# A fused attention and expert kernel: gates, own products and the last weight pieces take other places in the written order, and the late weight halves change engine

## What is computed

```
mag = sqrt(a_re^2 + a_im^2); scale = min(mag, 0.999) / (mag + 1e-6)
S = (a * scale) * S + outer(k[t], v[t])        # complex, per batch and head
y[t] = q[t] @ real(S)
xn = x / sqrt(mean(x^2) + 1e-6) * rms_g
x = (silu(xn @ w_gate) * (xn @ w_val)) @ w_out # 384 -> 1536 -> 384
expert = argmax(normalized(x) @ normalized(emb).T / tau)
out = gate * relu(x @ w1[expert]) @ w2[expert]
```

## Time and profile before

| | before |
|---|---|
| median of 3 runs | 1297.83 us (1294.12 to 1298.23) |
| profiled execution | 1298.23 us, span 1296.5 us |
| tensor engine busy | 1176.7 us, 91% |
| vector engine busy | 793.2 us, 61% |
| scalar engine busy | 616.1 us, 48% |
| GpSimd busy | 355.0 us, 27% |
| mean granted clock of the tensor engine | 0.977 |

### The profile page before, as it was taken

How to read it: one execution, slowest core, us unless ns; L and a number is a source line. 1 busy time by engine, 2 the same in 40 slices (tenths; PEclk the granted TensorE clock), 3 DMA queues, 4 the chain that set the end, 5 groups by cost and what they waited for, 6 DMA issues and landing times. The chain is left out here.

```text
span 1296.5 us, 46197 instructions
## 1 busy us (share of the span) xinstructions
PE 1176.7 (91%) x20003; PEld 1025.5 (79%) x20003; DVE 793.2 (61%) x1551; ACT 616.1 (48%) x1322; POOL 355.0 (27%) x345
## 2 busy tenths in 40 slices
PE   1778999899999999899999999899978999999995
PEld 0456879687887869687787969688848999999995
DVE  5886858586766858576675858444117555545553
ACT  4766463654636463564536374443322344333342
POOL 7131341333315041332405042300003132322221
PEclk9889999999999999999999999999998999999998
DMA  6221320210203020210203020000006633433310
GB/s 158 63 63 39 100 63 15 45 33 21 57 3 75 4 63 15 45 34 15 63 3 72 6 45 9 21 9 9 8 13 181 229 109 125 143 126 136 131 38 29
DMA packets 153380, 78.35 MB, mean 60 GB/s; under 512 B 130715, under 2 KB 144571, under 8 KB 153200
## 3 DMA queue, kind: packets, MB, share of 16 engines
q1 hardware_dynamic: 144800, 59.04, 17.2%
q0 software_dynamic: 4384, 11.88, 3.1%
q10 hardware_dynamic: 4016, 4.73, 1.0%
HBM read 66.15 MB, written 11.06 MB: 60 GB/s over the span
## 5 line engine op out<-in xcount | busy, mean ns | idle before, releaser
L965 PE MATMUL pO<-wo_sb,hid 128*128 128x384 f32 x576 | 207.3, 499 | 11.6 <-issue 11.0
L771 ACT ACTIVATE silu<-pGV 128x256 f32<-128x256 f32 x144 | 55.1, 383 | 260.6 <-PE pGV L953 260.1
L965 PEld LDWEIGHTS pO<-wo_sb,hid 128*128 128x128 f32 x576 | 104.0, 193 | 70.1 <-issue 15.5
L951 PE MATMUL pGV<-xT_hi,wg_hi 128*128 128x256 f32 x432 | 134.0, 310 | 0.7 <-DVE hid L619 0.4
L619 DVE TENSOR_TENSOR hid<-silu,pGV 128x256 f32<-128x256 f32 x144 | 58.5, 413 | 115.5 <-ACT silu L771 115.1
L1275 ACT ACTIVATE h_hi<-pH 128x256 fp32r<-128x256 f32 x128 | 49.1, 384 | 164.7 <-PE pH L1220 164.7
L952 PE MATMUL pGV<-xT_lo,wv_hi 128*128 128x256 f32 x432 | 121.6, 282 | 0.0
L953 PE MATMUL pGV<-xT_hi,wg_lo 128*128 128x256 f32 x432 | 121.6, 281 | 0.0
L951 PE MATMUL pGV<-xT_hi,wv_hi 128*128 128x256 f32 x432 | 121.6, 281 | 0.0
L952 PE MATMUL pGV<-xT_lo,wg_hi 128*128 128x256 f32 x432 | 121.5, 281 | 0.0
L953 PE MATMUL pGV<-xT_hi,wv_lo 128*128 128x256 f32 x432 | 121.5, 281 | 0.0
(11 more groups left out here) (230 smaller groups left out, 3081.9 us busy)
## 6 DMA issues: line engine op xcount, KB each, us to landing
w_sb<-in_moe_w SPq DMA_DIRECT2D x18, 1536.0 KB, 10.4
re<-in_a_re SPq DMA_DIRECT2D x24, 192.0 KB, 2.8
im<-in_a_im SPq DMA_DIRECT2D x24, 192.0 KB, 3.9
qin<-in_q SPq DMA_DIRECT2D x24, 192.0 KB, 2.8
kin<-in_k SPq DMA_DIRECT2D x24, 192.0 KB, 3.3
vin<-in_v SPq DMA_DIRECT2D x24, 192.0 KB, 3.7
routed_rows<-x ACTq DMA_DIRECT2D x24, 192.0 KB, 2.0
wo_sb<-in_moe_w_gate SPq DMA_DIRECT2D x3, 768.0 KB, 6.2
```

The costliest lines, as they stand in the source:

```text
L951: mm.matmul(to, hi, x_hi[:, kk, :], start=(kk == 0), stop=False)
L965: ins = mm.matmul(pO[:, 0:HD], hid[:, f, s_ * P:(s_ + 1) * P], wo_sb[:, f, :], start=(f == 0), stop=(f == NF - 1))
```

## The change

It has three parts. In `STEPS`, gate 2 stands ahead of the two squares and level 0 instead of behind level 0 and the route; own 0 stands ahead of gate 11 instead of behind level 6; sines 0, rotate 0 and own 1 stand right behind level 6, ahead of the first output parts. In `ONE_STEPS`, the four warm steps are gone; pieces 14 to 17 are done among the turns instead of among levels 0 to 2; every gate stands earlier, gates 0 and 1 ahead of level 0; own and sines stand in the places they have in `STEPS`, except that own 0 stands behind level 6. And the high and low halves of pieces 14 to 17 are made on the vector engine (`late_high`, `late_low`, with semaphores of their own), not on the scalar engine.

```diff
+ALL_PIECES, PIECES_AHEAD = 6 * KC, 14
 STEPS = [
...
-    ("lev", "turn", 10), ("lev", "turn", 11), ("lev", "first", 1), ("pre", "recip", 1), ("pre", "quotients", 1),
+    ("lev", "turn", 10), ("lev", "turn", 11), ("lev", "first", 1), ("pre", "recip", 1), ("pre", "quotients", 1), ("glu", "gate", 2),
     ("fin", "square", 0), ("fin", "square", 1),
-    ("lev", "level", 0), ("fin", "route", 0), ("glu", "gate", 2), ("glu", "gate", 3), ("pre", "tangent", 0), ("pre", "tangent", 1),
+    ("lev", "level", 0), ("fin", "route", 0), ("glu", "gate", 3), ("pre", "tangent", 0), ("pre", "tangent", 1),
...
-    ("lev", "level", 5), ("fin", "logits", 0), ("glu", "gate", 11),
-    ("lev", "level", 6), ("pre", "own", 0), ("finA", "out", 0), ("finA", "out", 1),
-    ("lev", "turn_back", 0), ("pre", "sines", 0), ("pre", "rotate", 0), ("pre", "own", 1), ("finA", "out", 2), ("lev", "turn_back", 1), ("pre", "sines", 1), ("pre", "rotate", 1), ("finA", "out", 3),
+    ("lev", "level", 5), ("fin", "logits", 0), ("pre", "own", 0), ("glu", "gate", 11),
+    ("lev", "level", 6), ("pre", "sines", 0), ("pre", "rotate", 0), ("pre", "own", 1), ("finA", "out", 0), ("finA", "out", 1),
+    ("lev", "turn_back", 0), ("finA", "out", 2), ("lev", "turn_back", 1), ("pre", "sines", 1), ("pre", "rotate", 1), ("finA", "out", 3),
 ONE_STEPS = [
+    ("lev", "turn", 0), ("lev", "turn", 1), ("glu", "norm", 0), ("wts", "late_high", 14), ("lev", "turn", 2), ("lev", "turn", 3), ("wts", "split", 14),
+    ("wts", "late_high", 15), ("lev", "turn", 4), ("lev", "turn", 5), ("glu", "scale", 0), ("wts", "late_low", 14),
+    ("wts", "late_high", 16), ("lev", "turn", 6), ("lev", "turn", 7), ("lev", "first", 0), ("wts", "split", 15), ("glu", "turn_in", 0),
+    ("wts", "late_high", 17), ("wts", "late_low", 15), ("lev", "turn", 8), ("lev", "turn", 9), ("wts", "split", 16), ("glu", "gate", 0), ("wts", "late_low", 16),
+    ("lev", "turn", 10), ("lev", "turn", 11), ("lev", "first", 1), ("next", "squares", 0), ("next", "squares", 1), ("wts", "split", 17), ("glu", "gate", 1), ("next", "signs", 0),
+    ("wts", "late_low", 17), ("next", "abs", 0), ("next", "abs", 1),
+    ("lev", "level", 0), ("next", "signs", 1), ("pre", "roots", 0), ("pre", "roots", 1), ("glu", "gate", 2), ("pre", "sums", 0),
+    ("lev", "level", 1), ("pre", "sums", 1), ("glu", "gate", 3), ("glu", "gate", 4), ("pre", "recip", 0),
+    ("lev", "level", 2), ("pre", "quotients", 0), ("glu", "gate", 5), ("glu", "gate", 6), ("pre", "recip", 1), ("pre", "quotients", 1),
+    ("lev", "level", 3), ("pre", "tangent", 0), ("pre", "tangent", 1), ("pre", "double", 0), ("pre", "double", 1), ("glu", "gate", 7), ("glu", "gate", 8),
+    ("lev", "level", 4), ("pre", "angle", 0), ("pre", "angle", 1), ("glu", "gate", 9), ("glu", "gate", 10),
+    ("lev", "level", 5), ("pre", "phase", 0), ("glu", "gate", 11),
+    ("lev", "level", 6), ("pre", "phase", 1), ("pre", "own", 0), ("pre", "own", 1), ("finA", "out", 0), ("finA", "out", 1),
+    ("lev", "turn_back", 0), ("pre", "sines", 0), ("pre", "rotate", 0), ("finA", "out", 2), ("lev", "turn_back", 1), ("pre", "sines", 1), ("pre", "rotate", 1), ("finA", "out", 3),
+    ("lev", "output", 0), ("lev", "output", 1), ("lev", "products", 0), ("lev", "state", 0), ("sq", "squares", 0), ("sq", "squares", 1),
+    ("finA", "out", 4), ("finA", "out", 5), ("sq", "signs", 0), ("sq", "signs", 1),
...
@@ sync
-                    sp.wait_ge(sm["wlo_ready"], 2 * 3 * KC)
+                    sp.wait_ge(sm["wlo_ready"], PIECES_AHEAD)
+                    sp.wait_ge(sm["wlo_late"], ALL_PIECES - PIECES_AHEAD)
@@ vector
+                            elif step == "late_high":
...
+                                dve.wait_ge(staged[n % 3], (n // 3 + 1) * 16)
+                                w.tensor_scalar((wg_hi, wv_hi)[n % 2][:, kk, part], landing[n % 3][:, kk, :], gcol[:, kk:kk + 1], None, ALU.mult
+                                                ).then_inc(sm["whi_late"], 1)
+                            elif step == "late_low":
...
+                                dve.wait_ge(sm["wdiff_ready"], x + 1)
+                                w.tensor_copy((wg_lo, wv_lo)[n % 2][:, kk, part], difference(x)).then_inc(sm["wlo_late"], 1)
@@ tensor, split
-                                pe.wait_ge(sm["whi_ready"], x + 1)
-                                if x > PIECES_AHEAD:
-                                    pe.wait_ge(sm["wlo_ready"], x)
-                                elif x >= 2:
+                                if x < PIECES_AHEAD:
+                                    pe.wait_ge(sm["whi_ready"], x + 1)
+                                else:
+                                    pe.wait_ge(sm["whi_late"], x + 1 - PIECES_AHEAD)
+                                if 2 <= x < PIECES_AHEAD:
                                     pe.wait_ge(sm["wlo_ready"], x - 1)
+                                elif x > PIECES_AHEAD:
+                                    pe.wait_ge(sm["wlo_late"], x - PIECES_AHEAD)
@@ tensor, gate
-                                    pe.wait_ge(sm["wlo_ready"], 2 * (f * 3 // NF + 1) * KC)
+                                    pe.wait_ge(sm["wlo_ready"], min(2 * (f * 3 // NF + 1) * KC, PIECES_AHEAD))
+                                if m == 0 and f == 2 * NF // 3:
+                                    pe.wait_ge(sm["wlo_late"], ALL_PIECES - PIECES_AHEAD)
```

More of the change, by code:

```diff
@@ L131 @@
 ONE_STEPS = [
[L132 to L145, removed]
@@ L146 @@
-    ("lev", "turn_back", 1), ("pre", "sines", 0), ("pre", "rotate", 0), ("finA", "out", 1), ("finA", "out", 2), ("lev", "output", 0), ("lev", "output", 1), ("pre", "sines", 1), ("pre", "rotate", 1), ("lev", "products", 0),
-    ("lev", "state", 0), ("sq", "squares", 0), ("sq", "squares", 1), ("finA", "out", 3), ("finA", "out", 4), ("finA", "out", 5), ("sq", "signs", 0), ("sq", "signs", 1),
+    ("lev", "turn", 0), ("lev", "turn", 1), ("glu", "norm", 0), ("wts", "late_high", 14), ("lev", "turn", 2), ("lev", "turn", 3), ("wts", "split", 14),
@@ L251, in build @@
             pM = ps(a, "pM", [P, 512])
-            names = ("wo_loaded a_cleared masks_ready scales_ready whi_ready wdiff_ready wlo_ready xhi_ready small_loaded sq_ready m2_ready turns_ready mag_ready a1_ready den_ready rm_ready "
+            names = ("wo_loaded a_cleared masks_ready scales_ready whi_ready wdiff_ready wlo_ready whi_late wlo_late xhi_ready small_loaded sq_ready m2_ready turns_ready mag_ready a1_ready den_ready rm_ready "
                      "signed_ready dd_ready rd_ready ima_ready rmd_ready t_ready r_ready rr_ready absre_ready at_ready th_ready "
@@ L279, in halves, with difference @@
                 return x[:, :, :].rearrange("p h t -> p (h t)").rearrange("p (n two l) -> p n two l", two=2, l=L)[:, :, side, :]
+            def difference(x):
+                return (pGV[x % 2] if x < PIECES_AHEAD else pO)[:, 0:THIRD]
             def pipeline(eng, body):
@@ L756, in body @@
                                 act.wait_ge(sm["wdiff_ready"], x + 1)
-                                s.activation((wg_lo, wv_lo)[n % 2][:, kk, part], (pGV[x % 2] if x < PIECES_AHEAD else pO)[:, 0:THIRD], ACT.Copy).then_inc(sm["wlo_ready"], 1)
+                                s.activation((wg_lo, wv_lo)[n % 2][:, kk, part], pGV[x % 2][:, 0:THIRD], ACT.Copy).then_inc(sm["wlo_ready"], 1)
                             elif step == "output" and x % 2:
@@ L813, in body @@
                                 pe.wait_ge(staged[n % 3], (n // 3 + 1) * 16)
-                                pe.wait_ge(sm["whi_ready"], x + 1)
-                                if x > PIECES_AHEAD:
-                                    pe.wait_ge(sm["wlo_ready"], x)
-                                elif x >= 2:
-                                    pe.wait_ge(sm["wlo_ready"], x - 1)
-                                mm.matmul((pGV[x % 2] if x < PIECES_AHEAD else pO)[:, 0:THIRD], times_g[kk], landing[n % 3][:, kk, :], start=True, stop=False)
-                                mm.matmul((pGV[x % 2] if x < PIECES_AHEAD else pO)[:, 0:THIRD], minus[:, :], (wg_hi, wv_hi)[n % 2][:, kk, part],
-                                          start=False, stop=True).then_inc(sm["wdiff_ready"], 1)
+                                if x < PIECES_AHEAD:
[3 more added lines that the diff above has]
+                                if 2 <= x < PIECES_AHEAD:
+                                    pe.wait_ge(sm["wlo_ready"], x - 1)
+                                elif x > PIECES_AHEAD:
+                                    pe.wait_ge(sm["wlo_late"], x - PIECES_AHEAD)
+                                to = difference(x)
+                                mm.matmul(to, times_g[kk], landing[n % 3][:, kk, :], start=True, stop=False)
+                                mm.matmul(to, minus[:, :], (wg_hi, wv_hi)[n % 2][:, kk, part], start=False, stop=True).then_inc(sm["wdiff_ready"], 1)
                             if step == "names_turned":
```

5 lines of the change are left out of this document (4 added, 1 removed).

## The result

| | before | after |
|---|---|---|
| median, 5 runs each on one chip | 1297.83 us (1292.96 to 1298.88) | 1305.91 us (1304.58 to 1310.14) |
| profiled execution | 1298.23 us, span 1296.5 | 1301.46 us, span 1299.6 |
| mean granted clock, profiled execution | 0.977 | 0.970 |

The ratio is 1.0079, with a 95% interval of 1.0051 to 1.0106. The time lies inside the range of the prediction, but the case it called likeliest, no difference, did not happen.

What follows compares the result with a forecast made beforehand. The tensor engine is fullest (68.6 of 73.3 us in a plain pass), so time lies in its idle places. Terms 3.6 - 6.0 + 3.6 = +1.2 on 1298.23 give 1299.4 us; range 1293.9 to 1301.7, wider 1290 to 1307.

Steps and rivals of the forecast that it cites:

- no difference: Whole kernel: time within 0.3%, 1293.9 to 1301.7 us, about what a measurement can't tell from no change; chance 0.50.
- Part 1, +3.6 us: Level 1, second chunk, plain passes: gate 2's multiply ahead in the vector queue delays it 0.4 us, nine times: +3.6 us.
- Part 2, -6.0 us: Outputs of passes 2 to 10: earlier own and sines remove the second chunk's output wait behind the state, -6.0 us.
- Part 3, +3.6 us: Pass 1: removed warming is spent on waiting, the vector engine's added copies delay level 0; +3.6 us, bounds -5.3 and +8.
- the walk: Pass 1 order followed with estimated lengths: level 0 on the vector engine near 123.4 against 115.17, level 6 7.3 us later.
- (a): Port, at the state's decay: both multiplies of rotate 1 hold it off, the wait stays, 6.0 us back, 1305.4; chance 0.10.
- (b): Clock in pass 1: three more half clock stretches, 1.7 us each, give +5 us, 1304.5; chance 0.22.
- (c): Pass 1 gains: the vector chain keeps up, so part 3 is -5.3 us, 1290.5; chance 0.13.
- (e): Part 1 in the plain passes costs nothing, the rest as forecast: 1295.8 us; chance 0.07.
- (d): Pauses where the second chunk's loads are issued move off: the 7.4 us before L928 gone, 1292.0; chance 0.08.

Runs made afterwards that it cites:

- e1_gate2: Kernel before with only gate 2 moved ahead of level 0 in the plain passes (part 1); ratio 1.0090 to before, median 1307.56 us.
- e2_own: Kernel before with only part 2: own 0 ahead of gate 11, sines 0, rotate 0 and own 1 right behind level 6; ratio 0.9948, median 1288.44 us.
- e4_one: Kernel before with only part 3: new pass 1 order and late weight halves on the vector engine; ratio 1.0012, median 1296.25 us.
- The filling matmul: Kernel before with part 1 plus one unused 128 x 384 matmul ahead of level 1 in every plain pass; ratio 1.0074 to before, median 1301.73 us.
- k4_one_order: Kernel before with part 3, but gate 1 and the last low half behind level 0 of pass 1; ratio 1.0002 to before, median 1293.37 us.

## Why the prediction was wrong, step by step

**Part 1, +3.6 us: the mechanism right, the term too small.** The place (level 1, second chunk), the cause (0.4 us in the vector queue), and the wait (1.34 us in pass 2; 11.2 us in the list of the kernel after, 12.4 in e1_gate2's) are as written. The step that failed is "level 1 starts about 0.4 us later [...] nine times: +3.6 us", with its upper bound of 0.5 for each: e1_gate2 is 12.5 us slower. 4.4 of them are the wait; up to 7.9 go with a granted clock of 0.9740 in place of 0.9801, with half clock granted right behind that wait in two of the nine passes. Pass 11, costed at nothing, has no such wait in e1_gate2 either. I had weighed the clock in pass 1 alone and priced a longer wait in passes 2 to 10 at its length. With 12.5 in place of 3.6 the sum would have been 1298.23 + 10.1 = 1308.3 us, against 1305.9 measured.

**Part 2, -6.0 us: right.** e2_own gave 0.9948, which is 6.7 us. The reduction fitted in its hole, the state's wait went, and the wait ahead of the first output part stayed (8.5, now 8.9; 9.9 in e2_own).

**Part 3, +3.6 us: the walk right in its places and too short for pass 1, the term not decided.** Level 0 on the vector engine was put between 122 and 125, and came at 121.67; counted from the pass's start that is 24.5 us against 15.0, 9.5 later where 8.2 was walked. The copies took 0.47 and 0.68 us (0.47 and 0.7 written), two of the splits' waits for low halves 1.52 and 0.75. The pass was put at 83 to 87 us, 84.6 by the sum, and took 87.65. Most of these 3 us are there by level 6, which came 9.9 us later in its pass than before, where 7.3 was walked. Of that difference 1.3 lie ahead of level 0 and 1.2 between level 0 and level 6, a way that the walk had 0.8 us shorter than before and that was 0.4 longer. But e4_one against before is 1.0012, +1.6 us, with an interval from -1.6 to +4.8, which holds the forecast and nothing at all.

**The rivals.** (a) The decay got its turn after one multiply (1.79 us) and ended before the second did; the wait did not come back. The Trainium skill's page "SBUF — State Buffer" (section "SBUF: two separate sides") has a vector operation with two SBUF inputs and a GpSimd operation that reads SBUF contend for one shared port pair, which the one that starts first holds for its whole instruction; QT, KT and the decay, 1.43 to 1.79 us beside a GpSimd multiply where level 0's QT takes 0.68 and the decay's median in before is 0.61, agree with it. (b) Half clock in pass 1: it came as written, at 98.98 to 105.81, 126.28 to 133.11 and 153.6 to 157.0, 17.1 us where before has 6.8, as much more as the three stretches of the rival. The tensor engine's work in pass 1 came to 74.2 us where my walk had 69.4. But e4_one, whose pass 1 has it too, is slower by 1.6 us, at most 4.8, and not by 3.6 + 5, so this rival is not what decided. That the times of (a) and (b), 1305.4 and 1304.5, lie near the measured 1305.9 is chance. (c) and (e) are refuted by 87.65 us and by 1.0090. (d) The pauses did not go; L928's have 7.8 us where 7.4 were, those at the levels grew from 1.7 to 5.4 us, and those before the outputs fell from 5.8 to 0.9.

**What stays open.** Why half clock follows some of the waits at level 1 and not others, and why 0.4 us more of each makes it so much more frequent. The filling matmul brought the clock back, but it is work itself, so only 3.4 of the 12.5 us came back, with intervals that overlap. No run changes the clock and leaves the wait, so the split of the 12.5 us between the two stays a sum of estimates. Where pass 1's loss went in the time of e4_one is open too. And the whole, 1.0079, is 0.3% more than the parts' sum, within the intervals; its clock, 0.967, is near what the parts' own drops give together (0.980 less 0.0061, 0.0008 and 0.0039 is 0.969).

## What to carry to other kernels

Ask of each step moved in a list that all engines share what it puts in front of on the engine that is already late at the next seam: 0.4 us on the vector engine ahead of level 0 cost 0.9%, 2.5 us taken out there gained 0.7%, and the same move without that one multiply cost nothing. Give such an engine an order of its own, and never put an operation that still waits for its input ahead of a chain that doesn't need it (2.04 us of waiting, 2.1% of time). And don't price a recurring wait of the busiest engine at its length alone while its clock can be granted lower: in the two cases here the mean time lost was 2.8 and 1.7 times the waits that grew.

## What was not expected of the hardware

A pause without any semaphore behind it, 3.39 us with 8 of 64 matmuls left, lay while w_out's load kept the DMA engines full (share 1.06, 395 GB/s, in the window above), and shrank from 3.10 to 1.20 us when that load was held back. The 6.83 us of half clock from 126.28 on begin with it. The load alone doesn't make it: in k4_one_order, where w_out's load was issued at 125.67, the pauses at the levels of pass 1 come to 0.5 us, and with the load held to 137.99 a pause of 1.20 us remained at the old place.

The mean granted clock of a kernel's timed runs falls by 0.006 to 0.008 with a few tenths of a microsecond to some two microseconds more of waiting in each pass. In a profile the rounded clock of the whole stretch hides this (0.99 in passes 2 to 10 of both kernels); the half clock stretches themselves show it, 6.8 us in before, 13.7 in after, 17.1 in e1_gate2.
